# A router matrix transposed by TensorE, a later pick of the first expert, two weight loads under way, and a shorter expert loop, in a fused attention + MoE kernel

## The reference

```python
x = attention(q, k, v)                       # 2304 x 512
y = (sigmoid(x @ w_gate) * (x @ w_val)) @ w_out      # width 1536
logits = y @ wr                              # wr is 512 x 8
expert = argmax(logits, axis=1); gate_w = softmax(logits)[expert]
for e in range(8):                           # rows of expert e only
    out[rows_e] = gate_w * (relu(y[rows_e] @ w1[e]) @ w2[e])    # 512 -> 1024 -> 512
```

## Time and profile before

| | |
|---|---|
| median of 3 runs | 955.5 us (955.02 to 957.89) |
| the profiled execution: its own time | 956.7 us |
| its span, first to last instruction | 955.0 us |
| PE busy | 888.4 us, 93% of the span |
| DVE, ACT, POOL busy | 465.8, 299.4, 220.1 us |
| mean granted TensorE clock | 0.974 of full speed |

### The profile page before, as it was taken

How to read it: one execution, slowest core, us unless ns; L and a number is a source line. 1 busy time by engine, 2 the same in 40 slices (tenths; PEclk the granted TensorE clock), 3 DMA queues, 4 the chain that set the end, 5 groups by cost and what they waited for, 6 DMA issues and landing times.

```text
span 955.0 us, 15676 instructions
## 1 busy us (share of the span) xinstructions
PE 888.4 (93%) x5198; PEld 734.7 (77%) x5199; DVE 465.8 (49%) x1082; ACT 299.4 (31%) x694; POOL 220.1 (23%) x233
## 2 busy tenths in 40 slices
PE   7989898990999999999999999999998999999995
PEld 3545454470899999999999999899987888888883
DVE  5777776730212533443533542675484445583261
ACT  5555554420323112112211311213333334362140
POOL 4123325320211211211111211131212223222121
PEclk9999999995899999999999999999999999999998
DMA  4544554457632000100200200114426345382110
GB/s 138 158 155 159 157 190 154 139 43 31 87 136 76 2 1 10 57 1 0 67 1 1 67 1 1 34 42 145 133 78 253 131 132 193 125 293 71 44 44 28
DMA packets 52199, 85.37 MB, mean 89 GB/s; under 512 B 13351, under 2 KB 25639, under 8 KB 52008
## 3 DMA queue, kind: packets, MB, share of 16 engines
q1 hardware_dynamic: 42272, 69.32, 24.2%
q0 software_dynamic: 3360, 10.50, 3.3%
q10 hardware_dynamic: 6504, 4.74, 3.1%
HBM read 70.30 MB, written 14.78 MB: 89 GB/s over the span
## 4 chain that ended last, share of the span: by engine, by line
PE 80%; DMA 9%; DVE 5%; issue 3%; ACT 1%; SPq 1%; POOL 0%; DVEq 0%; POOLq 0%; ACTq 0%
PE bank L1450 22%; PE bank L1452 22%; PE bank L1451 22%; PE bank L1422 3%; DMA woraw<-in_w_out 3%; PE bank L1383 3%; PE bank L1395 3%; DMA rinv_scratch<-rinv 3%; DMA rwide<-rinv_scratch 2%; PE bank L1592 2%; DVE nmax L1008 1%; PE bank L1555 1%; DMA yg<-y_scratch,gcol 1%; DVE xo L987 1%; ACT prob L815 1%
## 5 line engine op out<-in xcount | busy, mean ns | idle before, releaser
L1450 PE MATMUL bank<-xh,w1h 128*128 128x384 f32 x576 | 193.7, 336 | 0.0
L1452 PE MATMUL bank<-xh,w1l 128*128 128x384 f32 x576 | 193.1, 335 | 0.0
L1451 PE MATMUL bank<-xl,w1h 128*128 128x384 f32 x576 | 192.8, 335 | 0.0
L714 POOL TENSOR_TENSOR hl<-hraw,hh 128x384 fp32r<-128x384 f32 x72 | 83.7, 1163 | 397.3 <-ACT hh L844 397.3
L1197 DVE TENSOR_TENSOR hraw<-hraw,bank 128x384 f32<-128x384 f32 x72 | 39.9, 554 | 226.8 <-ACT hraw L889 226.3
L1450 PE MATMUL bank<-woh,hh 128*128 128x512 f32 x216 | 85.3, 395 | 27.4 <-POOL hl L714 27.4
L1450 PEld LDWEIGHTS bank<-xh,w1h 128*128 128x128 f32 x576 | 108.2, 188 | 2.4
L1451 PEld LDWEIGHTS bank<-xl,w1h 128*128 128x128 f32 x576 | 108.2, 188 | 2.2
L1452 PEld LDWEIGHTS bank<-xh,w1l 128*128 128x128 f32 x576 | 108.1, 188 | 0.0
L889 ACT ACTIVATE hraw<-bank 128x384 f32<-128x384 f32 x72 | 35.4, 492 | 225.9 <-PE bank L1452 225.9
L815 ACT ACTIVATE prob<-bank,nmax 128x576 f32<-128x576 f32 (+2 forms) x144 | 76.0, 529 | 88.7 <-DVE nmax L1008 86.3
(11 more groups left out here) (197 smaller groups left out, 1379.3 us busy)
## 6 DMA issues: line engine op xcount, KB each, us to landing
stage<-in_we SPq DMA_DIRECT2D x56, 512.0 KB, 4.9
w1raw<-in_w SPq DMA_DIRECT2D x8, 768.0 KB, 4.6
kt<-in_kT SPq DMA_DIRECT2D x16, 288.0 KB, 3.4
qt<-in_qT SPq DMA_DIRECT2D x16, 288.0 KB, 3.8
rwide<-rinv_scratch SPq DMA_DIRECT2D x32, 144.0 KB, 3.0
xt_scratch<-xo SPq DMA_DIRECT2D x16, 288.0 KB, 2.2
xraw<-xt_scratch SPq DMA_DIRECT2D x6, 768.0 KB, 4.9
y_scratch<-yrow ACTq DMA_DIRECT2D x6, 768.0 KB, 5.0
```

Of the source, the lines that this page charges most:

```text
L714: pool.tensor_tensor(hl[:, f % 2, :], hraw[:, f % 2, :], hh[:, f % 2, :].bitcast(F32), ALU.subtract).then_inc(h_low, 1)
L1450: pe.matmul(out_, wh, ah, start=first, stop=False, skip_group_check=True)
L1451: pe.matmul(out_, wh, al, start=False, stop=False, skip_group_check=True)
L1452: return pe.matmul(out_, wl, ah, start=False, stop=last, skip_group_check=True)
```

## The change

Four things change.

- The transposing DMA of ACT goes. PE turns `wr_sb` in four transposes in group 0 behind down(0, 1) (`turn_router`), DVE copies the result from PSUM, SP stores its 8 rows to `wrt_dram` and loads `wrb` one chunk later than before.
- `first_expert` moves from group 4, step 10, to group 5, step 0; `first_rows(0)` moves from step 0 to step 1; the logits of the last group take 0, 3, 6, 6, 6, 3 reductions in steps 0 to 5 (3, 3, 6, 6, 6 before).
- In `load(l)` SP waits before transfer k until transfer k-2 has landed, so that at most two weight loads are under way.
- The loop over pairs of loads ends at the last pair in use (`pairs`, a new entry of `ltab`, one more register load and a branch), and PE, DVE and POOL read their other values from `ltab` ahead of the loop instead of behind it.

```diff
         def route_steps(G):
             if G == G_LAST:
-                return [0, 3, 6, 12, 18, 24], 5, 6, 7, 8
+                return [0, 0, 3, 9, 15, 21, 24], 5, 6, 7, 8
...
-        WRB_STEP = 8
+        WRT_STEP, WRB_STEP = 3, 8
...
-            with eng.Fori(1, E // 2) as m:
-                load(2 * m, 0)
-                load(2 * m + 1, 1)
+            pairs = eng.value_load(ltab[0:1, 3 * NL + 3:3 * NL + 4], min_val=1, max_val=E // 2)
+            with eng.If(pairs > 1):
+                with eng.Fori(1, pairs) as m:
+                    load(2 * m, 0)
+                    load(2 * m + 1, 1)
...
                 if k == WRB_STEP:
+                    sp.wait_ge(wrt_out, 1)
+                    sp.dma_start(wrt_dram, yT[0:E].rearrange("p c n -> p (c n)")).then_inc(wrt_stored, 16)
+                if k == WRB_STEP + 1:
                     sp.wait_ge(wrt_stored, 16)
...
                         low_wait(sp, l - 1, k)
                         apart(sp)
+                    if k >= 2:
+                        sp.wait_ge(st_loaded[k - 2], 16 * l + 16)
+                        apart(sp)
+                    elif not (isinstance(l, int) and l == 0):
+                        sp.wait_ge(st_loaded[k + 6], 16 * l)
+                        apart(sp)
...
-            act.dma_start(wrt_dram, wr.rearrange("d e -> e d"), allow_slow_non_contiguous=True).then_inc(wrt_stored, 16)
...
+                    if first and f == WRT_STEP + 1:
+                        dve.wait_ge(wrt_done, 1)
+                        dve.tensor_copy(yT[0:E].rearrange("p c n -> p (c n)"), bank[3][0:E, 1, :]).then_inc(wrt_out, 1)
...
                         if f == 0 and G >= 2:
+                            if G - 2 == G_FIRST:
+                                first_expert()
                             add_table(G - 2)
-                            if G - 2 == G_FIRST:
-                                first_rows(0)
+                        if f == 1 and G - 2 == G_FIRST:
+                            first_rows(0)
...
             pe.wait_ge(loads_known, 1)
-            over_loads(pe, first_step, step, step)
             tiles = pe.value_load(ltab[0:1, 3 * NL + 1:3 * NL + 2], min_val=1, max_val=NT)
             last_load = pe.value_load(ltab[0:1, 3 * NL + 2:3 * NL + 3], min_val=0, max_val=E - 1)
+            over_loads(pe, first_step, step, step)
...
+            def turn_router():
+
+                pe.wait_ge(wr_loaded, 16)
+                for c in range(C):
+                    ins = pe.transpose(bank[3][0:E, 1, c * P:(c + 1) * P], wr_sb[:, c, :], ident[:])
+                ins.then_inc(wrt_done, 1)
```

More of the change, by code:

```diff
@@ L77, in bass_attention_ffn_moe @@
         logits = sb(ctx, "logits", [P, TT, E])
-        ltab = sb(ctx, "ltab", [P, 3 * NL + 3], I32)
+        ltab = sb(ctx, "ltab", [P, 3 * NL + 4], I32)
         lfirst = sb(ctx, "lfirst", [P, 2], I32)
@@ L271, in bass_attention_ffn_moe @@
         wrb_loaded = sem("wrb_loaded")
+        wrt_done = sem("wrt_done")
+        wrt_out = sem("wrt_out")
         wrt_stored = sem("wrt_stored")
@@ L786, in _ @@
             pool.wait_ge(loads_known, 1)
+            tiles = pool.value_load(ltab[0:1, 3 * NL + 1:3 * NL + 2], min_val=1, max_val=NT)
             over_loads(pool, step, step, step)
-            tiles = pool.value_load(ltab[0:1, 3 * NL + 1:3 * NL + 2], min_val=1, max_val=NT)
             scatter(tiles)
@@ L1221, in group @@
                             gates(G - 1)
-                            if G - 1 == G_FIRST:
-                                first_expert()
                         if f == tab_step + 1:
@@ L1274, in load_table @@
                 done(dve.tensor_scalar(ltabf[:, 3 * NL + 2:3 * NL + 3], used[:, E - 1:E], -1.0, None, ALU.add))
-                done(dve.tensor_copy(ltab[:], ltabf[:]))
+                done(dve.tensor_copy(ltab[:, 0:3 * NL + 3], ltabf[:]))
+                done(dve.tensor_scalar(ltab[:, 3 * NL + 3:], ltab[:, 3 * NL:3 * NL + 1], 1, None, ALU.arith_shift_right))
                 dve.sem_inc(loads_known, 1)
@@ L1353, in _ @@
             dve.wait_ge(loads_known, 1)
+            tiles = dve.value_load(ltab[0:1, 3 * NL + 1:3 * NL + 2], min_val=1, max_val=NT)
             over_loads(dve, first_step, second_step, lambda l, par, t: hidden(t), rest)
-            output(dve.value_load(ltab[0:1, 3 * NL + 1:3 * NL + 2], min_val=1, max_val=NT))
+            output(tiles)
         @block.tensor
@@ L1538, in group @@
                         down(G, f - 2)
+                    if first and f == WRT_STEP:
+                        turn_router()
                     if not first and f == route_steps(G)[2]:
```

## The result

| | before | after |
|---|---|---|
| median of the runs compared | 956.32 us (955.02 to 957.89, 4 runs) | 919.89 us (917.8 to 920.82, 4 runs) |
| profiled execution: its own time | 956.7 us | 919.3 us |
| span | 955.0 us | 917.6 us |
| mean granted TensorE clock | 0.974 | 0.993 |

The ratio is 0.9615, with a 95% interval of 0.9591 to 0.9639: the changed kernel is 3.9% faster. The forecast was 922.0.

The account below looks back on a forecast made before the run. PE fills 93% of the span, so its few gaps, chiefly 26.4 us ahead of down(0, 0), were taken as the bound. Terms -27.9 + 0.5 - 1.05 - 2.0 - 2.1 - 1.6 = -34.2 gave 922.5 or 921.3, stated 922.0, range 919 to 926.

Parts of the forecast that it names:

- The router: Between up(0, 2) and down(0, 0): without the element DMA PE's wait goes, -27.9 us; four added PE transposes cost +0.5.
- Rival 3: Ahead of down(0, 0): the router's DMA is not what held woraw and the wait stays, 949.9 us; chance 0.03.
- nothing else moved there: Argument against another cause of late woraw: no other transfer in that stretch, 0.02 MB taking 34.3% of the engines.
- The first expert: Group 4, step 11: moving its 17 operations to group 5 removes PE's gap, -1.05 us, at no cost there.
- Two loads under way: Gather behind the first expert: lands in 5.1 to 5.7 us instead of 7.7, -2.0 of PE's 3.0 us gap.
- Rival 1: Same gather as slow as before, one busy queue sufficing whatever its depth; 2.0 not gained, 924.0 us; chance 0.22.
- The rule of the Trainium skill that was weighed: DMA engines take turns between queue rows, a packet at a time, so limiting SP to two loads would gain the gather nothing.
- Rival 4: Expert loop: with two loads under way weights come too late and PE waits at each expert, 956 us or more; chance 0.01.
- The loop: Ahead of the last down: with register loads ahead of the loop PE restarts at 937.0 instead of 939.12, -2.1 us.
- The clock at the end: Last down: a shorter gap ahead of it keeps the full clock, -1.6 us.
- Rival 2: Last down: the clock falls all the same, since transposes ahead keep PE lightly used, 923.6 us; chance 0.12.
- the stall: PE's idleness ahead of down(0, 0), behind late woraw loads, taken as 26.4 us from one profile.

Follow-up runs that it names:

- s1_router: The kernel before with the router's part alone (PE transposes, DVE copy, SP store, no element DMA): 926.35 us, ratio 0.9631.
- a1_elem: The kernel after plus ACT's DMA of 4096 single elements at its old place, into a tensor nothing reads: 954.44 us, ratio 0.9901.
- a3_flat: The kernel after plus an ACT DMA of the same 16 KB in eight contiguous runs, into a tensor nothing reads: 923.62 us, ratio 0.9593.
- a4_all: The kernel after without the limit of two, so four weight loads are issued at once again: 923.67 us, ratio 0.9613.
- s3_two: The kernel before with at most two weight loads under way, alone: 957.8 us, ratio 0.9953.
- a5_one: The kernel after with at most one weight load under way in place of two: 921.0 us, ratio 0.9558.
- a6_pairs: The kernel after with the bounded loop, but PE, DVE and POOL reading their last values behind the loop again: 916.76 us, ratio 0.9536.
- a7_ahead: The kernel after with values read ahead of the loop, but the loop again going through three pairs, the last empty: 924.07 us, ratio 0.9606.
- s2_first: The kernel before with only the first expert moved to group 5 and the logits shifted: 959.14 us, ratio 0.9992.
- a0_after: The kernel after run again unchanged, as base on another chip: 919.06 us, ratio 0.9541.

## Why the prediction held, point by point

*The router* (-27.9 and +0.5). From up(0, 1) to up(0, 3) the traces differ by 28.07 us, and s1_router confirms that this part does it alone. The four transposes cost 0.43: down(0, 1) to down(0, 2) takes 6.70 us after, where all other such steps take 6.27. The mechanism, that single elements hold back what is issued behind them, was argued from one row; a1_elem to a3_flat show it for the loads and stores on SP's queue; of other queues that stretch says nothing. Rival 3 falls. One argument against it was wrong all the same: "nothing else moved there" overlooks SP's own stores of x, one of them issued at 208.88. The flat copy, with the same stores beside it, leaves no gap.

*The first expert* (-1.05). The gap went and none came. It was worth 1.3 by s1_router against after (458.97 and 457.68 us from the first up to the last down). The term was read as idleness, which is counted from the modelled end of the matmul before; by starts, the two at that gap in s1_router are 1.45 apart (579.44 and 580.89) and the next 0.31, where 0.23 is the pace, so 1.3. The product of step 2 was 0.7 late, not 1.3, and ACT was held 0.30, not 2 us; both cost nothing, as forecast.

*Two loads under way* (-2.0). The landing of 4.7 lies below the 5.1 to 5.7 assumed, so the gap shrank by 2.7, and 0.42 of it came back at the next gather, 0.4 more in small steps behind it. Net 1.9; a4_all says 1.8 to 2.0. The sum was right with two errors against each other: the forecast looked at one gather and didn't ask what the spread loads do to the next. Rival 1 falls by s3_two, a4_all and a5_one: the depth of SP's queue is what counts. The rule of the Trainium skill that was weighed, turns between queue rows ("DMA: Bandwidth & Descriptors", "Queues, rings and completion order"), does not by itself describe these rows: gap 2.70 with four under way, 0.31 with two, none with one. What in the chip makes depth count, no run here shows. Rival 4 falls too: in the waits of after, and of a5_one, PE waits for no weights.

*The loop* (-2.1) was 1.98, the gap 3.13 to 1.15. The prediction charged the gap to the empty pair's four register loads and the two behind the loop together. a6_pairs shows that taking away the four is enough; a7_ahead, that taking away the two alone gives 1.32 of it.

*The clock at the end* (-1.6) came as forecast, but the reason was half right. Of five profiles with a last gap of 1.81 or more, four show the fall; of nine with 1.15, none. The long gap goes with the fall, it doesn't settle it (s2_first). Rival 2 falls for the gap of 1.15.

*What was not forecast* is the clock in routing, 1.6 us, and attention, 1.3. From the y transposes to `turn_rows(2)` before took 22.50 us and after 20.93. The windows of before, then of after: us, PE, PEld, DVE, ACT and POOL busy (instructions), clock, DMA share, GB/s:

```profile
691.00:694.00 3.00, 3.00 (x8) 2.40 (x8) 2.55 (x14) 0.75 (x2) 0.00 (x0) 0.53 0.01 3
```

```profile
661.00:664.00 3.00, 3.00 (x16) 2.48 (x15) 2.43 (x13) 0.82 (x2) 0.00 (x0) 1.00 0.01 3
```

Four of fourteen profiles show that fall, with the change (a4_all, a5_one) and without it (before, s3_two). So it comes with the change and without it, as by a draw, though fourteen profiles can't exclude that the odds differ. One kernel's own executions differ in the same way: the mean granted clock of a7_ahead was 0.986, 0.992, 0.988 and 0.993 in its four runs. Attention's difference is no part of the change either, by the spread of 194.3 to 200.5. These two make 2.9 of the 3.2 us between the forecast for the profiled execution, 922.5, and its 919.3. They are luck, not the change; without them the sum is met within 0.3 us.

One thing in the forecast was too narrow: the stall was taken as 26.4 us. The same DMA, and its copy in a1_elem, held PE for 26.36, 28.56, 32.08, 33.69 and 36.30 us in five profiles. Before's times range from 953 to 974 and after's from 918 to 922 (a0_after's included). On the chip of a0_after the ratio was 0.9541, a gain of 46 us where the forecast had 34. That the forecast came so close is in part luck: before's profile, from which the term was taken, has the shortest stall of the five, and the four runs of before beside it, 955.02 to 957.89, are from the low end of that range.

## What to carry to other kernels

A short transfer in a queue is judged by its number of pieces, not by its bytes: 16 KB in 4096 elements held PE for 26 to 36 us, and as eight contiguous runs for none. When a DMA lands late, look at what else was issued just before it, on any queue, and then hold back how many large transfers are under way where a small one that PE needs comes behind them. Ahead of a last short piece of work, count what the sequencer has to go through (empty rounds of a loop, register loads): here it made 2.0 us of a gap of 3.13. And compare kernels by the stretch that was changed when the stretch ahead of it varies by more than the gain.

## What the runs showed of the hardware that was not expected

- An element-wise DMA issued on ACT's queue delays the loads issued on SP's: from the issue of the elements to PE's restart 38.4 us (before) to 48.4 (a1_elem, 204.91 to 253.29) for 4096, 30.9 for 2048 (202.23 to 233.13), and 11.9 with the flat copy, where nothing is held. That is 26.5 to 36.5 us for 4096 elements and 19.0 for 2048, an estimate of 6.5 to 9.3 ns for each, from one profile of each kernel. The Trainium skill, "DMA: Bandwidth & Descriptors", "Rules for kernel authors", says that a non-contiguous last dimension makes one descriptor per element and should be avoided; the packets (4103, 2052, 32) agree, and the price for other queues is what these runs add. Why the same DMA holds PE for 26 us at one time and 36 at another stays open.
- The lower clock does not come at fixed places: routing, with no gap ahead of it, lost 1.6 us in four profiles of fourteen, and behind the gather gap of 2.7 to 3 us it fell in s2_first alone (2.8 us) of five profiles that have it. The window of 717 to 720 us there shows the granted clock as 0.50, which is 1.2 of 2.4 GHz:

```profile
717.00:720.00 3.00, 3.00 (x9) 2.32 (x9) 0.69 (x1) 0.59 (x1) 0.36 (x2) 0.50 1.02 419
```

  The Trainium skill, "TensorE: Matmul & The Clock Gate", Part 1, has the monitor behind the clock run freely, not started by the kernel. That would make such draws; no run here shows it, as none sets where the kernel starts against the monitor.
- A gather of the same 128 rows landed in 4.7 us (5.1 in s3_two) with at most two loads under way, in 7.7 beside four, and in 3.5 at the median of before's 22. Two under way did not always give 4.7: the next one in after took 6.6.
